# Two fused feed-forward layers: chunk pairs 0 and 1 of the second layer in slots of 14 half-height matmuls a side, and the first tile's split taken earlier from PSUM

## What is computed

```python
def _attn_ref(x, weight_gen):          # x: 2 x 4096 x 192, weight_gen: 2 x 4096 x 8 x 7
    w = softmax(weight_gen, axis=-1)
    # causal convolution of 7 taps; each of 8 heads weighs its 24 columns
    out = np.einsum('bshk,bskhg->bshg', w, x_unf)
...
h = np.maximum(x @ w_in, 0.0)          # 192 -> 2048
x = h * h @ w_out                      # 2048 -> 192
...
h = x @ w_in                           # 192 -> 2048
g = h * np.cos(h)
return g @ w_out                       # 2048 -> 192
```

## Time and profile before

| what | value |
|---|---|
| median of 3 runs | 1176.79 us (1176.7 to 1177.63) |
| the profiled execution, its own time | 1176.98 us |
| its span | 1175.2 us |
| PE busy | 1167.0 us, 99% |
| PEld busy | 1127.6 us, 96% |
| DVE busy | 962.0 us, 82% |
| ACT busy | 806.2 us, 69% |
| POOL busy | 367.3 us, 31% |
| chain that ended last | PE 94%, POOL 3%, DVE 1%, ACT 1%, issue 1% |

### The profile page before, as it was taken

The page is one execution under the profiler, slowest core; times in us unless marked ns, Lnnn a source line. Parts: engine busy times, 40 slices in busy tenths (PEclk is TensorE's granted clock), DMA queues, the critical chain, the costliest instruction groups (busy, mean ns, idle before and its releaser), DMA issues.

```text
span 1175.2 us, 25694 instructions
## 1 busy us (share of the span) xinstructions
PE 1167.0 (99%) x9906; PEld 1127.6 (96%) x9906; DVE 962.0 (82%) x1505; ACT 806.2 (69%) x1468; POOL 367.3 (31%) x265
## 2 busy tenths in 40 slices
PE   9999999999999999999999999999999999999998
PEld 7989999999999999999999999999999999999987
DVE  7978898878778787887878878787787878878787
ACT  5877766666667676666766666676666766666676
POOL 4994634070420606125070430705215070000000
PEclk9999999999999999999999999999999999999999
DMA  8511111110111101111111111101111000100001
GB/s 211 138 51 29 37 27 35 25 33 12 23 35 29 35 11 18 35 28 35 17 22 29 25 35 28 35 9 21 35 29 35 13 17 3 26 2 15 1 1 28
DMA packets 113173, 37.32 MB, mean 32 GB/s; under 512 B 101662, under 2 KB 110878, under 8 KB 113052
## 3 DMA queue, kind: packets, MB, share of 16 engines
q1 hardware_dynamic: 111100, 34.87, 14.1%
q10 hardware_dynamic: 1952, 0.80, 0.3%
HBM read 23.84 MB, written 6.29 MB: 26 GB/s over the span
## 4 chain that ended last, share of the span: by engine, by line
PE 94%; POOL 3%; DVE 1%; ACT 1%; issue 1%; SPq 0%; DMA 0%; POOLq 0%; DVEq 0%; ACTq 0%
PE y L608 49%; PE h L608 44%; POOL wd_lo L564 1%; POOL wa_lo L562 1%; POOL wo L568 1%; POOL wo L566 0%; DVE tap L1428 0%; DMA xc<-in_x_dram 0%; POOL gen L548 0%; ACT relu L1142 0%; DVE xd_lo L1533 0%; ACT gen L1131 0%; SPq L392 0%; DVE tap L1435 0%; PE y L674 0%
## 5 line engine op out<-in xcount | busy, mean ns | idle before, releaser
L608 PE MATMUL y<-g_hi,wo 64*128 64x512 f32 x3048 | 693.8, 393 | 0.2
L608 PE MATMUL y<-g_lo,wo 64*128 64x512 f32 x2032 | 514.8, 392 | 0.0
L608 PEld LDWEIGHTS y<-g_hi,wo 64*128 64x128 f32 x3048 | 412.8, 184 | 14.8 <-PE y L608 1.5
L529 POOL TENSOR_TENSOR tap<-xc,gen 128x768 f32<-128x768 f32 x98 | 150.9, 1546 | 575.2 <-DVE xd_lo L1515 555.1
L608 PEld LDWEIGHTS y<-g_lo,wo 64*128 64x128 f32 x2032 | 297.4, 184 | 2.2
L1167 ACT ACTIVATE turns<-turns 128x512 f32<-128x512 f32 x238 | 150.2, 631 | 182.5 <-DVE turns L1466 182.5
L608 PE MATMUL h<-xa_hi,wa_hi 64*128 64x512 f32 x1018 | 266.5, 396 | 0.2 <-issue 0.2
L608 PE MATMUL h<-xa_hi,wa_lo 64*128 64x512 f32 x1018 | 261.9, 391 | 0.0
L608 PE MATMUL h<-xa_lo,wa_hi 64*128 64x512 f32 x1018 | 261.5, 391 | 0.0
L1486 DVE TENSOR_TENSOR h<-h,turns 128x512 f32<-128x512 f32 x238 | 165.6, 696 | 114.7 <-ACT turns L1167 114.2
L1460 DVE SCALAR_TENSOR_TENSOR h<-h,relu 128x512 f32<-128x512 f32 x249 | 173.3, 696 | 55.9 <-ACT relu L1142 53.4
(11 more groups left out here) (125 smaller groups left out, 1075.1 us busy)
## 6 DMA issues: line engine op xcount, KB each, us to landing
xc<-in_x_dram SPq DMA_DIRECT2D x60, 240.0 KB
out_dram<-arena SPq DMA_DIRECT2D x62, 64.0 KB, 1.9
xt_a<-x_blocks SPq DMA_DIRECT2D x224, 16.0 KB, 1.8
arena<-in_moe_w_out_dram SPq DMA_DIRECT2D x16, 192.0 KB, 3.6
arena<-in_moe_w_in_dram SPq DMA_DIRECT2D x16, 128.0 KB, 2.7
out_dram<-arena SPq DMA_DIRECT2D x62, 32.0 KB, 1.7
xt_d<-x_blocks SPq DMA_DIRECT2D x112, 16.0 KB, 1.8
arena<-in_moe_w_in_dram SPq DMA_DIRECT2D x16, 64.0 KB, 3.4
```

Of the source, the lines that this page charges most:

```text
L529: pool.tensor_tensor(tap[:, k % 2, :].rearrange("p (r g) -> p r g", g=GROUP), rows[k], wk, ALU.mult).then_inc(pool_step, 1)
L608: return pe.matmul(o, w[rows, :], x[rows, :], start=start, stop=stop)
```

## The change

Four things change.

- PE: slot 17's second down projection is no longer five full-height matmuls but ten halves (`catch_down`), both sides, with the waits between the sides.
- PE: slots 19 and 20 (m = 0 and 1) run a new `opening_slot`: first layer's up, second layer's up and one down projection, 14 halves on each side. `h2_left` is now counted from chunk 0 on, so every wait for it is one higher.
- ACT and DVE: the first tile's split stands in slot 17 right behind `relu` of chunk 17 (ACT) and its square (DVE), ahead of chunk 17's high and low part. The sum of part d is written back to PSUM (`y2`), and its high and low part are taken from there. The dummy sine moves behind slot 17.
- ACT: pieces 12 to 15 are rounded from slots 19, 21, 23 and 25 on instead of 15, 18, 20 and 22.

```diff
-        HI_AT = {4: 2, 5: 4, 6: 5, 7: 6, 8: 8, 9: 9, 10: 11, 11: 13, 12: 15, 13: 18, 14: 20, 15: 22}
+        HI_AT = {4: 2, 5: 4, 6: 5, 7: 6, 8: 8, 9: 9, 10: 11, 11: 13, 12: 19, 13: 21, 14: 23, 15: 25}
...
-        SIN_AFTER = 16
+        SIN_AFTER = 17
...
-            return n + 1 - (n > CATCH_UP - D1)
+            return n + 1
...
+        def y1_d_sum(t):
+
+            return first_sums(0)[DD:P, 1, :] if t == 1 else y1_part
...
-                if m <= 0:
+                if m in range(D2):
+                    opening_slot(n, m, par, of, o1, o2, f1, f2, down1)
+                    return
+
+                if m < 0:
                     head_slot(t, i, par, o1, down1)
                     if n == CATCH_UP:
...
-                        down_alone(*down_at(k)).then_inc(down1_done, 1)
-                    if m == 0:
-                        pe.wait_ge(x2_split, 1)
-                        up_alone(o2, 1, f2, of).then_inc(up2_done, 1)
+                        catch_down(n - D1)
                     return
...
+            def catch_down(k):
+
+                down = down_at(k)
+                pe.wait_ge(g1_ready, k + 1)
+                pe.wait_ge(y1_d_done, k)
+                down_d(down, TOP, 0)
+                pe.wait_ge(down1_done, k)
+                down_a(down, BOTTOM, 0)
+                down_d(down, TOP, 1).then_inc(y1_d_left, 1)
+                down_a(down, BOTTOM, 1)
+                down_a(down, BOTTOM, 2).then_inc(y1_a_left, 1)
+                pe.wait_ge(y1_d_left, downs_in_halves(k))
+                down_d(down, BOTTOM, 0)
+                pe.wait_ge(y1_a_left, downs_in_halves(k))
+                down_a(down, TOP, 0)
+                down_d(down, BOTTOM, 1, stop=True).then_inc(y1_d_done, 1)
+                down_a(down, TOP, 1)
+                down_a(down, TOP, 2, stop=True).then_inc(down1_done, 1)
+
+            def opening_slot(n, m, par, of, o1, o2, f1, f2, down):
...
+                up_d(o1, 0, f1, par, 2).then_inc(h1_left, 1)
+                up_d(o2, 1, f2, of, 2).then_inc(h2_left, 1)
+                pe.wait_ge(h2_left, m + 1)
+                up_a(o2, 1, f2, of, TOP, 0)
+                pe.wait_ge(g1_ready, k + 1)
+                pe.wait_ge(down1_done, k)
+                down_a(down, BOTTOM, 0, start=True)
+                up_a(o2, 1, f2, of, TOP, 1)
+                down_a(down, BOTTOM, 1)
+                up_a(o2, 1, f2, of, TOP, 2, stop=True).then_inc(up2_done, 1)
+                down_a(down, BOTTOM, 2).then_inc(y1_a_left, 1)
+                pe.wait_ge(y1_d_done, k)
+                down_d(down, TOP, 0, start=True)
+                pe.wait_ge(h1_left, n - HEAD_D1 + 1)
+                up_a(o1, 0, f1, par, BOTTOM, 0)
+                down_d(down, TOP, 1).then_inc(y1_d_left, 1)
+                up_a(o1, 0, f1, par, BOTTOM, 1)
+                pe.wait_ge(y1_a_left, downs_in_halves(k))
+                down_a(down, TOP, 0)
+                up_a(o1, 0, f1, par, BOTTOM, 2, stop=True).then_inc(up1_done, 1)
+                down_a(down, TOP, 1)
+                pe.wait_ge(y1_d_left, downs_in_halves(k))
+                down_d(down, BOTTOM, 0)
+                down_d(down, BOTTOM, 1, stop=True).then_inc(y1_d_done, 1)
+                down_a(down, TOP, 2, stop=True).then_inc(down1_done, 1)
```

And in `slot` of ACT and of DVE:

```diff
+                if i == Y1_AT and t == 1:
+                    x2_part(t, par)
+                    x2_high_a(t, par)
+                    x2_high_d(t, par)
                 if live(n) and m != 0:
                     high(n)
...
+                if i == Y1_AT and t == 1:
+                    sum_y1(t)
+                    x2_low_a(t, par)
+                    x2_low_d(t, par)
                 if live(n) and m != 0:
                     low(n)
```

More of the change, by code:

```diff
@@ L652, in up_alone @@
                 return up_d(o, l, f, par, 2, stop=True)
[L654 to L664, removed]
             def last_down(k, y, l, f, hi, lo):
@@ L796, in last_tail_up @@
                 down_d(down, TOP, 0)
-                pe.wait_ge(h2_left, m)
+                pe.wait_ge(h2_left, m + 1)
                 up_a(o, 1, f, of, TOP, 0, cols)
@@ L806, in last_tail_up @@
                 down_a(down, BOTTOM, 2)
-                pe.wait_ge(h2_left, m + 1)
+                pe.wait_ge(h2_left, m + 2)
                 up_a(o2, 1, f, of, TOP, 0, cols2)
@@ new lines, in opening_slot @@
+            def opening_slot(n, m, par, of, o1, o2, f1, f2, down):
+                k = down_of_slot(n)
+                pe.wait_ge(g1_ready, before_in_bank(n) + 1)
+                if m % PF == 0:
+                    pe.wait_ge(piece_ready[PL + m // PF], 2)
+                up_a(o1, 0, f1, par, TOP, 0, start=True)
+                pe.wait_ge(x2_hi_ready, 1)
+                up_a(o2, 1, f2, of, BOTTOM, 0, start=True)
+                up_a(o1, 0, f1, par, TOP, 1)
+                up_a(o2, 1, f2, of, BOTTOM, 2)
+                up_a(o1, 0, f1, par, TOP, 2)
+                pe.wait_ge(y1_read, 1)
+                up_a(o2, 1, f2, of, BOTTOM, 1)
+                up_d(o1, 0, f1, par, 0)
+                pe.wait_ge(x2_split, 1)
+                up_d(o2, 1, f2, of, 0)
+                up_d(o1, 0, f1, par, 1)
+                up_d(o2, 1, f2, of, 1)
+                up_d(o1, 0, f1, par, 2).then_inc(h1_left, 1)
+                up_d(o2, 1, f2, of, 2).then_inc(h2_left, 1)
+                pe.wait_ge(h2_left, m + 1)
+                up_a(o2, 1, f2, of, TOP, 0)
[20 more added lines that the diff above has]
+                down_a(down, TOP, 2, stop=True).then_inc(down1_done, 1)
@@ L1180, in slot @@
                     act.activation(g2_hi[:, c, :], h2[c], ACT.Copy, scale=2.0 * math.pi).then_inc(g2_hi_ready, 1)
-                if i == Y1_AT and t == 1:
-                    x2_part(t, par)
-                    x2_high_a(t, par)
-                if i == y1_at(t) and 0 < t < TILES:
+                if i == y1_at(t) and 1 < t < TILES:
                     x2_high_d(t, par)
@@ L1218, in x2_high_d @@
                 act.wait_ge(y1_summed, t)
-                act.activation(xd_hi[DD:P, 1 - par, :], y1_part, ACT.Copy).then_inc(x2_hi_ready, 1)
+                act.activation(xd_hi[DD:P, 1 - par, :], y1_d_sum(t), ACT.Copy).then_inc(x2_hi_ready, 1)
                 if t == TILES:
@@ L1497, in slot @@
                                              ALU.subtract).then_inc(g2_ready, 1)
-                if i == Y1_AT and t == 1:
-                    sum_y1(t)
-                    x2_low_a(t, par)
-                if i == y1_at(t) and 0 < t < TILES:
+                if i == y1_at(t) and 1 < t < TILES:
                     x2_low_d(t, par)
@@ L1532, in x2_low_d @@
                 dve.wait_ge(x2_hi_ready, 2 * t)
-                dve.tensor_tensor(xd_lo[DD:P, 1 - par, :], y1_part, xd_hi[DD:P, 1 - par, :],
+                dve.tensor_tensor(xd_lo[DD:P, 1 - par, :], y1_d_sum(t), xd_hi[DD:P, 1 - par, :],
                                   ALU.subtract).then_inc(x2_split, 1)
```

9 lines of the change are left out of this document (2 added, 7 removed).

## The result

| | before | with the change |
|---|---|---|
| median | 1176.78 us (22 runs) | 1178.88 us (22 runs, 1178.56 to 1180.0) |
| ratio of medians | | 1.0016, 95% interval 1.0010 to 1.0023 |
| profiled execution, own time | 1176.98 us | 1178.85 us |
| its span | 1175.2 us | 1177.0 us |

The change makes the kernel 1.9 us longer by the profiled executions and 2.1 us by the medians. That is within 0.2% of before, as forecast, and on the side of the forecast. But the forecast was +0.9 us, less than half of what was measured, and 1178.88 us lies 0.08 us above the end of the range.

The account below looks back on a forecast made before the run. PE bounds the steady slots; in the opening, slot 21 waits for the ACT and DVE chain from relu of chunk 19. Opening +0.7 and late pieces +0.2 make +0.9 on the median 1176.79: 1177.7 us, range 1176.4 to 1178.8.

Parts of the forecast that it names:

- same within 0.2%: Whole kernel: a time within 0.2% (2.4 us) of before counts as the same; chance 0.91.
- Slot 17 in halves: Slot 17's second down projection: two hand-overs eat what pairs save; slot 18 starts at 63.93 instead of 63.56, +0.4 us.
- The split: Behind relu of chunk 17: xd_lo takes 0.69 us, but chunk 17's low part comes later; slot 19 +1.0 us.
- From slot 19 to slot 21: Chain from relu of chunk 19 at 70.57 takes 5.51 us to slot 21, which starts at 76.08.
- The opening's term: Opening, up to slot 21: slot 21 starts 0.7 us later than before, adding +0.7 us.
- Pairs in slots 19 and 20: 14 pairs a slot: slot 20 takes 3.7 us, and the PE saving becomes 1.5 us of waiting before slot 21.
- The rival in which PE sets the pace: Slot 21 starts when PE is ready, at 73.0 with 0.8 us for hand-overs: 1173.6 to 1174.4 us; chance 0.04.
- The late pieces: Piece operations last until slot 27 instead of 24: 3 x 0.07 = +0.2 us, bounds nothing and +0.4.
- Nothing arrives late: Piece 15's last operation moves by 13 us to about 111.5, ahead of its first need in slot 33 at 129.
- The lower clock: Rival: PE's idle before slot 21 halves the clock over one slot, another 4.4 us, 1182 us; chance 0.03.
- the early sums: Rival: slot 17's hand-overs overlap better, slot 19 starts at 66.6; 1176.7 to 1177.0 us; chance 0.18.
- The sum: Whole kernel: +0.7 us from the opening and +0.2 from the pieces, +0.9 us in all, median 1177.7 us.

Follow-up runs that it names:

- e4: Changed kernel with slot 17's second down projection at full height again (five matmuls): 1178.17 us, ratio 1.0011.
- e3: Changed kernel with the first tile's split back behind chunk 17's high and low part: 1177.91 us, ratio 1.0009.
- e5: Changed kernel with the second layer's chunk 0 ahead of chunk 19 on ACT and DVE in slot 19: 1177.65 us, ratio 1.0007.
- e7: Changed kernel with e1, e3 and e5 together: 1175.58 us, ratio 0.9991.
- e1: Changed kernel with pieces 12 to 15 back behind slots 15, 18, 20 and 22: 1177.95 us, ratio 1.0009.
- e2: Kernel before with only pieces 12 to 15 moved to slots 19, 21, 23 and 25: 1177.45 us, ratio 1.0006.
- e8: Changed kernel with pieces 12 to 15 two slots earlier, from slots 17, 19, 21 and 23 on: 1178.13 us, ratio 1.0009.
- e6: Kernel before with only the first tile's sum of part d written to PSUM and split from there: 1176.69 us, ratio 1.0000.
- e10: e7 with slot 17's second down projection at full height again: 1175.51 us, ratio 0.9989.

## Why the prediction was right, and why too small

The direction, the order of events in the opening and the "same within 0.2%" were right; the size was not, and one term accounts for most of the difference.

- **Slot 17 in halves.** Predicted: slot 18 at 63.93 and the hand-overs at 0.54 us each. Measured: 64.00. Right, and e4 shows what they cost on the path: 0.39 us at slot 18, 0.7 us in slot 21 and in the time.
- **The split.** Predicted: sum at 64.27, xd_lo at 65.71 in 0.69 us, chunk 17's low part ending at 67.12, slot 19 at 67.2. Measured: 64.37, 65.83 in 0.69, 67.25, 67.30. Right, each 0.1 late; e3 shows that the low part's place is the cause.
- **From slot 19 to slot 21.** Predicted: relu of chunk 19 at 3.37 behind slot 19, and 5.51 us from there to slot 21. Measured: 3.54, and 76.35 - 70.84 = 5.51. The 0.17 us are in the first pair (0.34 for 0.31), at the hand-over (the side that leads to relu goes on at 69.17, 0.59 behind 68.58, for 0.54), in the half behind it (0.30 for 0.23) and in ACT's reaction (0.44 for 0.42). The half that waits for h2_left itself starts at 69.07, only 0.49 behind. The chain from relu of chunk 19 was read right, and e5 shows that it decides. The opening's term was +0.7 and measured +0.92.
- **Pairs in slots 19 and 20.** Predicted: slot 20 takes 3.7 us and PE idles 1.5. Measured: slot 20 at 71.03, idle 1.41. Right. The rival in which PE sets the pace was given only 0.8 us for hand-overs and so had slot 21 at 73.0, 12.0 behind the anchor. e7 is that case, and there it is 12.83.
- **The late pieces: the step that failed.** "3 x 0.07 = +0.2 us; bounds are nothing and ... +0.4" measured -0.29 + 1.09 = +0.80. Both e1 and e2 show it as the pieces' own, e8 that it depends on where the last one ends. The step read a price per slot off slot 21 and added it for three slots more; with the change slots 22 to 25 pay no such price. What it left out is the debt, which came due as 1.09 us: an engine behind its time costs nothing until the next extra work comes, and the rows that show the slack, relu's 0.45 us of waiting in slot 28, were in the trace of before. "Nothing arrives late" was right and was not the question.
- **The lower clock** and **the early sums** did not come: the granted clock is 1.00 in the windows around slot 21, and slot 19 started at 67.30, not 66.6.
- **The sum.** +0.7 and +0.2 forecast, +0.92 and +0.80 measured. With the 0.07 us of the anchor that is the 1.8 us by which the spans differ. The medians differ by 2.1, 0.2 more by the profiled execution of before being 0.2 above its median, as the prediction noted; that of the change is not.

## What to carry to other kernels

Work moved off one engine's busy stretch is a debt on the engine that does it: before moving it, look up where that engine next waits (here 0.45 us in one slot of ACT) and what extra comes before it can wait again. When a change makes the bounding engine faster over a stretch, follow the chain behind it and reorder the followers too; the new slots gained nothing until turns of chunk 0 stood first. And an operation taken earlier on an in-order engine gains nothing when what it waits for has not moved, and delays all that it has passed.

## What the runs showed of the hardware

- DVE's xd_lo with both operands in SBUF took 2.07 us beside POOL's multiplication, with one in PSUM 0.69 (e6). The small operation on `stat` (TENSOR_SCALAR, 128x64, both sides in SBUF) takes 1.46 to 1.72 us beside POOL's convolution; it took 0.52 us at 55.45 in the trace of before, beside POOL's low parts of a piece. No experiment took POOL's work away, but the trace of before has both operations once more in a stretch where POOL does nothing (29.59 us up to 166.49), and there they take 0.69 and 0.18 us:

```profile
137.12 0.69 DVE L1533 TENSOR_TENSOR xd_lo<-y_part,xd_hi 64x512 fp32r<-64x512 f32 x1
...
160.23 0.18 DVE L1323 TENSOR_SCALAR stat<-stat 128x64 f32<-128x64 f32 x1
```

```profile
166.49 3.05 POOL L529 TENSOR_TENSOR tap<-xc,gen 128x768 f32<-128x768 f32 x2 [29.59 <-DVE xd_lo L1515]
```

- A hand-over between the two sides of the array cost about 0.3 us over running on: 0.54 to 0.55 us start to start in slot 17, 0.49 in slot 19 for the half that waits. Slots 19 and 20 have several. They took 3.76 and 3.67 us in e7, where 14 pairs would be 3.26.
- Changing from full height to half height cost about 0.1 us: slot 19 starts 2.52 us behind slot 18 with the full-height down projection ahead of slot 18 (e10), and 2.42 with halves (e7).
- The first weights arrive unevenly: the anchor lay between 60.84 and 62.31 us in 13 profiles. Absolute times past it, from two single profiles, can't be compared to better than that.
